# Making the taps' exponentials on GpSimd as powers of e in a fused dynamic convolution and SwiGLU kernel

## Chip, cores and metric

The kernel runs on one core of a Trainium2 chip. The metric is the device time of one execution in microseconds; the median of several runs is taken. The engines are named TensorE (PE in the profile, PEld its weight loads), VectorE (DVE), ScalarE (ACT), GpSimd (POOL) and SyncE (SP, which here only starts transfers).

## What is computed

The input x is 4 sequences of 4096 tokens with 192 numbers each; weight_gen has 8 heads of 7 taps for every token. The taps are made into weights by a softmax over the 7, and each token becomes a weighted sum of itself and the six tokens before it. The result goes through a gated MLP of width 1536.

```python
w = weight_gen - np.max(weight_gen, axis=-1, keepdims=True)
w = np.exp(w)
w = w / (np.sum(w, axis=-1, keepdims=True) + 1e-09)
...
out = np.einsum('bshk,bskhg->bshg', w, x_unf)
...
rms = np.sqrt(np.mean(x * x, axis=-1, keepdims=True) + 1e-06)
xn = x / rms * rms_g
g = xn @ w_gate
silu = g * (1.0 / (1.0 + np.exp(-g)))
val = xn @ w_val
return (silu * val @ w_out).astype(np.float32)
```

## The kernel before

Each of the 128 partitions holds 128 successive tokens. The work goes in 32 tiles (TILES) of 4 tokens per partition (J), 512 tokens in all. A tile's hidden layer is 12 blocks f of 128 rows. fp32 products are made in three parts from a rounded and a remaining half (w_hi, w_lo; xT part 0 and 1; h_hi, h_lo).

The order on each engine is written out by hand, with semaphores between the engines. In tile T:

- TensorE runs block f's gate and value products into PSUM (L620), and every two blocks the output projection of the two before (L651, L655). In the middle of the tile (block 5, for tile 0 block 9: `turn_after`, L154) it transposes the next tile's normalised input (L588, L592).
- ScalarE makes silu of the gate (L410) and, when VectorE has made h = value x silu (L544), the rounded h_hi (L417). Between these stand the squares of the next tile (L367, blocks 0 and 1), the scaling by 1/rms (L374, blocks 2 and 3), and the rounding of the transposed input (L379, L381). ScalarE works in order: a late scaling holds the silu behind it, and a late silu holds VectorE and TensorE.
- VectorE makes h (L544) and h_lo (L562) of each block. Between these stand the 17 steps of the convolution two tiles ahead (`mix`, L458): 4 of softmax normalising (L185 to L190, 32 or 224 columns), and 13 products and additions of 768 columns (L201, L203). Lists `steps_first`, `steps_taps` and `steps_other` (L528 to L530) say how many go with each block.
- GpSimd makes two small instructions per tile (`inverse_rms`, L289): an add (L292), and 1/rms as a power with exponent -0.5 (L294), each on 4 columns. At the start it also makes a part of tile 0's convolution and all of tile 1's.
- SyncE loads the inputs, moves halves of the transposed input between partitions (xT<-xT, L251) and stores results.

The taps of all tiles lie in one SBUF tensor, 224 columns per tile (32 token-heads of 7). Those of tiles 0 to FIRST-1 (FIRST is 3) are loaded first, in two pieces (`FIRSTS`): their maximum and difference are `less_max` on VectorE (L443), their Exp `first_exps` on ScalarE (L334). The others come in one transfer and are treated in three pieces, tiles 3 to 7, 8 to 19 and 20 to 31 (`cuts`, L163). Piece n has its maximum (`rest_maxima`, L506) and its difference (`rest_subtract`, L512) between VectorE's blocks of tile n, and its Exp (`rest_exps`, L389) on ScalarE behind block 9 of tile n. Exp and Silu lie in different tables of ScalarE, so each of these Exps has an ACT_TABLE_LOAD before it and one behind it. VectorE waits for the first piece's Exp at tile 1 and for all of them at tile 3 (L554). VectorE, ScalarE, GpSimd and SyncE run most tiles in loops (Fori) of two tiles; TensorE's tiles are written out.

Of the kernel before, what the change touches and what calls it, by code (L numbers as in the profile page):

```python
# [1 line left out]

# [3 lines left out]
ALU = mybir.AluOpType  # L6
ACT = mybir.ActivationFunctionType
AX_X = mybir.AxisListType.X
# [8 lines left out]
def dynconv_swiglu(nc, x, weight_gen, w_gate, w_val, w_out, rms_g, out):  # L17
# [18 lines left out]
    SLOTS = D // DB  # L36
    HB = 4
    CHUNKS = ((0, 1, 2), (1, 0, 2))
    FIRST = 3
    FIRSTS = ((0, 1), (1, FIRST))  # L40
    assert D == 192 and 2 * DB == P and F % P == 0 and (S // TOK) * TOK == S and TILES % 2 == 0
    NORM, CONV = 4, 2 * K - 1
# [9 lines left out]
    with ExitStack() as ctx:  # L52
        def sb(name, shape, dt=F32):
            return ctx.enter_context(nc.sbuf_tensor(name, shape, dt))
# [31 lines left out]
        mean_sq = sb("mean_sq", [P, J])  # L86
        minus_half = sb("minus_half", [P, J])
        eps_rms = sb("eps_rms", [P, J])
        zero = sb("zero", [P, 1])
        inv_rms = sb("inv_rms", [P, J])  # L90

# [68 lines left out]
            return f if f <= xf else f + 1  # L160


        cuts = [FIRST, 8, 20, TILES]  # L163
        pieces = [slice(a * J * H, b * J * H) for a, b in zip(cuts, cuts[1:])]

        def main_to(t, part):

# [111 lines left out]
        @block.gpsimd  # L279
        def _(pool):  # L280
            nc.gpsimd.memset(ident[:], 0.0).then_inc(pool_steps, 1)
            nc.gpsimd.memset(minus_half[:], -0.5).then_inc(pool_steps, 1)
            nc.gpsimd.memset(eps_rms[:], EPS_RMS).then_inc(pool_steps, 1)
            nc.gpsimd.memset(zero[:], 0.0).then_inc(pool_steps, 1)
            pool.wait_ge(pool_steps, 4)
            nc.gpsimd.affine_select(out=ident[:], in_=ident[:], compare_op=ALU.not_equal, fill=1.0, base=0,
                                    pattern=[[-1, P]], channel_multiplier=1).then_inc(consts_done, 1)

            def inverse_rms(T):  # L289

                pool.wait_ge(squared, J * (T + 1))
                nc.gpsimd.tensor_tensor(mean_sq[:], sq_mean[:], eps_rms[:], ALU.add).then_inc(mean_done, 1)  # L292
                pool.wait_ge(mean_done, T + 1)
                nc.gpsimd.tensor_tensor(inv_rms[:], mean_sq[:], minus_half[:], ALU.pow).then_inc(rms_done, 1)  # L294

            for b in range(2):
                p = b * (S // TOK)
                if b == 0:
                    pool.wait_ge(halo_loaded, 32)
                    pool.wait_ge(consts_done, 1)  # L300
                else:

                    pool.wait_ge(pool_zeroed, b)
                nc.gpsimd.memset(x_first[p:p + 1, 0:PAD, :], 0.0).then_inc(pool_zeroed, 1)
            pool.wait_ge(first_mix, NORM0_DONE)
            pool.wait_ge(pool_zeroed, 2)
            pool.wait_ge(x_zeroed, B - 2)
            pool.wait_ge(xfirst_loaded[0], 16)
            for n in range(CONV):
                if n:  # L310
                    pool.wait_ge(pool_mix, n)
                conv_step(nc.gpsimd, n, x_first[:, 0:PAD + J, :], tap_w, y[:, 0, :, :], prod_pool, J0, J).then_inc(pool_mix, 1)
            inverse_rms(0)
            pool.wait_ge(first_mix, NORM1_DONE)
            pool.wait_ge(xfirst_loaded[1], 16)
            for n in range(CONV):
                pool.wait_ge(pool_mix, CONV + n)
                conv_step(nc.gpsimd, n, x_first[:, J:PAD + 2 * J, :], tap_w1, y[:, 1, :, :], prod_pool).then_inc(pool_mix, 1)

            for T in range(1, 5):  # L320
                inverse_rms(T)

            def turn(i, last=False):
                for t in range(2):
                    if not (last and t == 1):
                        inverse_rms(2 * i + t + 1)

            with pool.Fori(2, TILES // 2 - 1) as i:
                turn(i)
            turn(TILES // 2 - 1, last=True)  # L330

        @block.scalar
        def _(act):
# [52 lines left out]
            act.wait_ge(wo_loaded, 16)  # L386
            nc.scalar.activation(wo[:, :, 0, :], raw_out, ACT.Copy).then_inc(w_hi_done, 1)

            def rest_exps(n):  # L389
                act.wait_ge(rest_less, n + 1)  # L390
                nc.scalar.activation(taps[:, pieces[n], :], taps[:, pieces[n], :], ACT.Exp).then_inc(rest_exp, 1)  # L391

            def out_low(T):


                act.wait_ge(bank_left, J * FB * (T + 1))
                nc.scalar.activation(out_part, out_ps[:, :, D:2 * D], ACT.Copy).then_inc(out_part_done, 1)  # L397

            def tile(T, t, first=False, last=False, exps=()):
                xf = turn_after(T)  # L400
                squares_at, scales_at = (xf - 4, xf - 3) if first else (0, 1), (xf - 2, xf - 1) if first else (2, 3)
                for f in range(FB):
# [23 lines left out]
                    for at, n in exps:  # L426
                        if f == at:
                            rest_exps(n)
# [13 lines left out]
        def _(dve):  # L442
# [63 lines left out]
            def rest_maxima(n):  # L506

                if n == 0:
                    dve.wait_ge(taps_loaded, 16)
                nc.vector.tensor_reduce(tap_max[:, pieces[n]], taps[:, pieces[n], :], AX_X, ALU.max).then_inc(rest_max, 1)  # L510

            def rest_subtract(n):  # L512

                dve.wait_ge(rest_max, n + 1)
                cols = pieces[n]
                nc.vector.tensor_tensor(taps[:, cols, :], taps[:, cols, :],
                                        tap_max[:, cols].unsqueeze(2).to_broadcast([P, cols.stop - cols.start, K]),
                                        ALU.subtract).then_inc(rest_less, 1)

            def out_add(T, t, stored):  # L520
                dve.wait_ge(out_part_done, T + 1)
# [4 lines left out]


            steps_first = [0, 0, 2, 2, 0, 2, 2, 2, 2, 2, 2, 1]  # L528
            steps_taps = [2, 2, 2, 0, 2, 2, 2, 0, 2, 1, 1, 1]
            steps_other = [2, 1, 2, 2, 1, 1, 1, 1, 2, 1, 2, 1]  # L530
            assert sum(steps_first) == sum(steps_taps) == sum(steps_other) == MIX

            def tile(T, t, i, first=False, mixes=True, last=False):
                xf = turn_after(T)
                tops = isinstance(T, int) and T < len(pieces)
                steps = steps_first if first else steps_taps if tops else steps_other
                max_at, subtract_at = (1, 4) if first else (3, 7)
                for f in range(FB):
                    b = pair(t, step_of(f, xf))
                    if f == 2 and not first:  # L540
                        out_add(T - 1, 1 - t, None if isinstance(T, int) and T < 3 else 16 * (i - (1 - t)))
                    dve.wait_ge(silu_done, FB * T + f + 1)
                    dve.wait_ge(val_done, FB * T + f + 1)
                    nc.vector.tensor_tensor(h[:, f % 2, :], val_ps[:, b, :], silu[:, f % 2, :], ALU.mult).then_inc(h_done, 1)  # L544
                    if first and f == 0:
                        wo_low()
                    if mixes:
                        for n in range(sum(steps[:f]), sum(steps[:f + 1])):
                            if n == 0:

                                dve.wait_ge(x_loaded[t], 16 * (i + 1))
# [17 lines left out]
            tile(0, 0, 0, first=True)  # L569
            tile(1, 1, 0)  # L570
            tile(2, 0, 1)
            tile(3, 1, 1)
            with dve.Fori(2, TILES // 2 - 1) as i:
                tile(2 * i, 0, i)
                tile(2 * i + 1, 1, i)
            tile(TILES - 2, 0, TILES // 2 - 1, mixes=False)
            tile(TILES - 1, 1, TILES // 2 - 1, mixes=False, last=True)
            out_add(TILES - 1, 1, 16 * (TILES // 2 - 1))

        @block.tensor  # L580
# [148 lines left out]
```

## Time and profile before

| | us |
|---|---|
| median of 3 runs | 1323.94 (1322.46 to 1326.7) |
| profiled execution | 1322.03 |
| its span in the trace | 1320.2 |
| TensorE busy | 1277.4 (97%) |
| VectorE busy | 992.0 (75%) |
| ScalarE busy | 662.8 (50%) |
| GpSimd busy | 83.3 (6%) |

The profile is that of one execution. Busy time is the time in which an engine's instructions run; matmuls are pipelined, so a busy TensorE needn't be at its peak. Idle time of an engine is put down to what released it: in a row, "[4.91 <-ACT silu L410]" says that the engine sat idle for 4.91 us until ScalarE's silu was there. The granted clock is TensorE's, as a share of 2.4 GHz. Times in rows are us from the span's start unless ns are named.

### The profile page before, as it was taken

Reading aid. Unit: us, or ns where it says so; the run is one execution under the profiler, and the core shown is the slowest. Engines: PE = TensorE matmul, PEld = TensorE weight load, DVE = VectorE, ACT = ScalarE, POOL = GpSimd, SP = SyncE. Lnnn points to the kernel's source line nnn. Section 1 sums busy time; section 2 is a strip of 40 time slices with the busy share of each in tenths; the row PEclk is TensorE's granted clock in tenths of the full one; section 3 lists DMA queues with packets and bytes.
Section 4 is the critical chain, followed back from the end, with each engine's and each line's share of the span. In section 5 each row is a group of like instructions: output and inputs, shape, how many; then the busy total and the mean of one; then the engine's idle time right before and its main releaser. Section 6 shows DMA issues by size and latency. Waiting matters only on the chain.

```text
span 1320.2 us, 33644 instructions
## 1 busy us (share of the span) xinstructions
PE 1277.4 (97%) x13524; PEld 1260.1 (95%) x13524; DVE 992.0 (75%) x1441; ACT 662.8 (50%) x1427; POOL 83.3 (6%) x101
## 2 busy tenths in 40 slices
PE   3798999999999999999999999999999999999998
PEld 3687889999999999999999999999999999999998
DVE  6788877777777778777778777777777777777653
ACT  4364565445555445555444555444555444555543
POOL 7600000000000000000000000000000000000000
PEclk9799999999999999999999999999999999999999
DMA  9121211211221211221211221111121121121010
GB/s 307 38 67 27 65 58 52 67 56 37 67 67 43 67 55 37 67 67 43 67 55 41 63 67 48 62 55 56 47 67 60 50 67 55 37 67 37 14 37 13
DMA packets 20101, 77.69 MB, mean 59 GB/s; under 512 B 3215, under 2 KB 5007, under 8 KB 19854
## 3 DMA queue, kind: packets, MB, share of 16 engines
q1 hardware_dynamic: 19982, 75.83, 18.9%
q8 instruction: 108, 1.77, 0.5%
q14 instruction: 11, 0.09, 0.0%
HBM read 38.07 MB, written 12.58 MB: 38 GB/s over the span
## 4 chain that ended last, share of the span: by engine, by line
PE 89%; DVE 5%; issue 2%; ACT 2%; DMA 1%; POOL 0%; SPq 0%; POOLq 0%
PE up_ps L620 59%; PE out_ps L651 26%; PE out_ps L655 3%; DVE y L203 1%; DVE h L544 1%; DVE h_lo L562 1%; DMA xT<-xT 1%; DVE prod L201 1%; PE up_ps L588 1%; ACT taps L391 0%; ACT silu L410 0%; PE up_ps L592 0%; DMA taps<-in_weight_gen 0%; ACT h_hi L417 0%; DVE y L201 0%
## 5 line engine op out<-in xcount | busy, mean ns | idle before, releaser
L620 PE MATMUL up_ps<-xT,w_hi 64*128 64x512 f32 x4608 | 858.1, 396 | 14.9 <-DMA xT<-xT 6.5
L620 PEld LDWEIGHTS up_ps<-xT,w_hi 64*128 64x128 f32 x4608 | 627.3, 186 | 26.1 <-issue 8.1
L620 PE MATMUL up_ps<-xT,w_lo 64*128 64x512 f32 x2304 | 589.2, 395 | 0.0
L651 PE MATMUL out_ps<-wo,h_hi 64*128 64x384 f32 x3072 | 478.2, 354 | 3.1 <-issue 2.7
L655 PE MATMUL out_ps<-wo,h_lo 64*128 64x192 f32 x3072 | 453.3, 247 | 0.0
L544 DVE TENSOR_TENSOR h<-up_ps,silu 128x512 f32<-128x512 f32 x384 | 264.7, 689 | 234.1 <-ACT silu L410 233.8
L651 PEld LDWEIGHTS out_ps<-wo,h_hi 64*128 64x128 f32 x3072 | 425.8, 185 | 5.1 <-issue 3.9
L655 PEld LDWEIGHTS out_ps<-wo,h_lo 64*128 64x128 f32 x3072 | 421.2, 187 | 0.5
L417 ACT ACTIVATE h_hi<-h 128x512 fp32r<-128x512 f32 x384 | 242.7, 632 | 352.3 <-DVE h L544 292.0
L410 ACT ACTIVATE silu<-up_ps 128x512 f32<-128x512 f32 x384 | 228.7, 595 | 263.7 <-PE up_ps L620 259.5
L620 PEld LDWEIGHTS up_ps<-xT,w_lo 64*128 64x128 f32 x2304 | 349.5, 187 | 3.3
L562 DVE TENSOR_TENSOR h_lo<-h,h_hi 128x512 fp32r<-128x512 f32 x384 | 265.2, 691 | 40.2 <-ACT h_hi L417 40.2
L203 DVE TENSOR_TENSOR y<-y,prod 128x768 f32<-128x768 f32 (+1 forms) x186 | 177.4, 954 | 2.1
L201 DVE TENSOR_TENSOR prod<-x_buf,tap_w 128x768 f32<-128x768 f32 x180 | 171.1, 951 | 1.5
L292 POOL TENSOR_TENSOR mean_sq<-sq_mean,eps_rms 128x4 f32<-128x4 f32 x32 | 8.2, 258 | 1149.2 <-ACT xn L367 1149.2
L374 ACT ACTIVATE xn<-y,inv_rms 128x128 f32<-128x128 f32 (+1 forms) x256 | 74.1, 360 | 4.4 <-POOL inv_rms L294 4.4
L525 DVE TENSOR_TENSOR last<-out_ps,last 128x768 f32<-128x768 f32 x32 | 30.6, 957 | 27.4 <-ACT last L397 27.4
L367 ACT ACTIVATE xn<-y 128x192 f32<-128x192 f32 x128 | 44.4, 348 | 1.6 <-DVE y L203 1.6
L294 POOL TENSOR_TENSOR inv_rms<-mean_sq,minus_half 128x4 f32<-128x4 f32 x32 | 34.0, 1064 | 2.5
L470 DVE TENSOR_TENSOR xT<-up_ps,xT 128x512 fp32r<-128x512 f32 x32 | 22.1, 691 | 10.7 <-ACT xT L381 9.2
L201 DVE TENSOR_TENSOR y<-x_buf,tap_w 128x768 f32<-128x768 f32 x30 | 28.7, 957 | 1.0
L473 DVE TENSOR_TENSOR xT<-up_ps,xT 64x256 fp32r<-64x256 f32 x64 | 26.6, 416 | 1.0
(43 smaller groups left out, 311.4 us busy)
## 6 DMA issues: line engine op xcount, KB each, us to landing
x_buf<-in_x SPq DMA_DIRECT2D x30, 960.0 KB, 4.5
xT<-xT SPq DMA_DIRECT2D x96, 256.0 KB, 3.8
result<-last SPq DMA_DIRECT2D x32, 384.0 KB, 2.3
taps<-in_weight_gen SPq DMA_DIRECT2D x1, 3248.0 KB, 19.5
raw<-in_moe_w_gate SPq DMA_DIRECT2D x3, 384.0 KB, 6.3
raw<-in_moe_w_val SPq DMA_DIRECT2D x3, 384.0 KB, 7.3
last<-in_moe_w_out SPq DMA_DIRECT2D x1, 1152.0 KB, 12.4
x_first<-in_x SPq DMA_DIRECT2D x2, 384.0 KB, 4.6
```

The lines of the kernel that those rows point to most:

```text
L201: return engine.tensor_tensor(heads(product if n else acc), heads(flat(src[:, k + j0:k + j1, :])), w[:, q0:q1, k].unsqueeze(2).to_broadcas ...
L203: return engine.tensor_tensor(acc, acc, product, ALU.add)
L294: nc.gpsimd.tensor_tensor(inv_rms[:], mean_sq[:], minus_half[:], ALU.pow).then_inc(rms_done, 1)
L367: nc.scalar.activation(xn[:, j * D:(j + 1) * D], y[:, t, j, :], ACT.Square, scale=D ** -0.5, accum_out=sq_mean[:, j:j + 1]).then_inc(squar ...
L374: nc.scalar.activation(part[:, j, :], y[:, t, j, d], ACT.Copy, scale=inv_rms[:, j:j + 1]).then_inc(xn_done, 1)
L410: nc.scalar.activation(silu[:, f % 2, :], gate_ps[:, b, :], ACT.Silu).then_inc(silu_done, 1)
L417: nc.scalar.activation(h_hi[:, f % HB, :], h[:, f % 2, :], ACT.Copy).then_inc(h_hi_done, 1)
L544: nc.vector.tensor_tensor(h[:, f % 2, :], val_ps[:, b, :], silu[:, f % 2, :], ALU.mult).then_inc(h_done, 1)
L562: nc.vector.tensor_tensor(h_lo[:, f % HB, :], h[:, f % 2, :], h_hi[:, f % HB, :].bitcast(F32), ALU.subtract).then_inc(h_lo_done, 1)
L620: mm = nc.tensor.matmul(ps[:, banks, :], w[rows, s, cols], xT[rows, t, s, part, :], start=(s == 0 and n == 0), stop=ends)
L651: nc.tensor.matmul(out_ps[:, j, 0:2 * D], h_hi[rows, g % HB, cols], wo[rows, g, :, :].rearrange("p a d -> p (a d)"), start=(g == 0 and k < ...
L655: mm = nc.tensor.matmul(out_ps[:, j, 0:D], h_lo[rows, g % HB, cols], wo[rows, g, 0, :], start=False, stop=(g == FB - 1 and k >= 2), skip_g ...
```

## The change

The taps of tiles 0 to 3 (FIRST is 4) keep ScalarE's Exp. For all others GpSimd makes the exponential as `pow` of a constant tensor filled with e and the differences, one instruction of 224 columns per tile. The maxima and differences on VectorE, before in pieces of 5 and 12 tiles, are made for tiles 4 to 7 in one go (maximum in tile 0 behind block 4, difference in tile 1 behind block 4), and from tile 8 on tile by tile, two tiles' worth in each of the tiles 3 to 14: maximum behind block 4 and difference behind block 6, and again behind blocks 7 and 9. GpSimd makes the powers of tiles 4 to 7 behind the inverse_rms it issues in tile 1, and two in each of the tiles 3 to 14 behind that tile's inverse_rms. VectorE waits for the power of tile T+2 before it normalises it in tile T. ScalarE has no table load between silus any more. The loops of VectorE, ScalarE and GpSimd are written out, and the list `steps_taps` goes (tiles 1 to 3 take `steps_other`).

```diff
-    FIRST = 3
+    FIRST = 4
...
+        euler = sb("euler", [P, J * H * K])
...
-        cuts = [FIRST, 8, 20, TILES]
-        pieces = [slice(a * J * H, b * J * H) for a, b in zip(cuts, cuts[1:])]
+        AHEAD = 8
+        def taps_at(T, f):
+
+            if T < 3 or f not in (4, 6, 7, 9):
+                return None
+            c = AHEAD + 2 * (T - 3) + f // 7
+            return c if c < TILES else None
...
+            nc.gpsimd.memset(euler[:], math.e).then_inc(pool_steps, 1)
+            pool.wait_ge(pool_steps, 5)
...
-            for T in range(1, 5):
-                inverse_rms(T)
...
+            def rest_exp_of(c):
+
+                pool.wait_ge(rest_less, c + 1 - FIRST)
+                w = taps[:, c * J * H:(c + 1) * J * H, :].rearrange("p q k -> p (q k)")
+                nc.gpsimd.tensor_tensor(w, euler[:], w, ALU.pow).then_inc(rest_exp, 1)
+
+            for T in range(TILES):
+                if T < TILES - 1:
+                    inverse_rms(T + 1)
+                if T == 1:
+                    for c in range(FIRST, AHEAD):
+                        rest_exp_of(c)
+                for f in (6, 9):
+                    c = taps_at(T, f)
+                    if c is not None:
+                        rest_exp_of(c)
...
-            def rest_exps(n):
-                act.wait_ge(rest_less, n + 1)
-                nc.scalar.activation(taps[:, pieces[n], :], taps[:, pieces[n], :], ACT.Exp).then_inc(rest_exp, 1)
...
-            tile(0, 0, first=True, exps=((9, 0),))
-            tile(1, 1, exps=((9, 1),))
-            tile(2, 0, exps=((9, 2),))
-            tile(3, 1)
-            with act.Fori(2, TILES // 2 - 1) as i:
-                tile(2 * i, 0)
-                tile(2 * i + 1, 1)
-            tile(TILES - 2, 0)
+
+            tile(0, 0, first=True)
+            for T in range(1, TILES - 1):
+                tile(T, T % 2)
...
-                                if isinstance(T, int) and T in (1, 3):
-
-                                    dve.wait_ge(rest_exp, 1 if T == 1 else len(pieces))
+                                if T + 2 >= FIRST:
+
+                                    dve.wait_ge(rest_exp, T + 3 - FIRST)
...
-                    if tops and f == max_at:
-                        rest_maxima(T)
-                    if tops and f == subtract_at:
-                        rest_subtract(T)
...
+                    if T == 0 and f == 4:
+                        rest_maxima(FIRST, AHEAD)
+                    if T == 1 and f == 4:
+                        rest_subtract(FIRST, AHEAD)
+                    c = taps_at(T, f)
+                    if c is not None:
+                        if f in (4, 7):
+                            rest_maxima(c, c + 1)
+                        else:
+                            rest_subtract(c, c + 1)
```

## Rows read from the trace of the kernel before

**Rows 1.** The page's first part: busy time, share of the span, instructions of each engine.
```profile
PE 1277.4 (97%) x13524; PEld 1260.1 (95%) x13524; DVE 992.0 (75%) x1441; ACT 662.8 (50%) x1427; POOL 83.3 (6%) x101
```

**Rows 2.** Stretches in us; busy us (instructions) by engine, PE's granted clock, DMA.
```profile
45.00:85.00 40.00, 36.03 (x372) 33.12 (x370) 35.47 (x45) 21.12 (x44) 12.19 (x7) 0.98 0.09 21
85.00:131.00 46.00, 42.37 (x428) 36.54 (x430) 37.09 (x49) 25.30 (x48) 1.21 (x2) 0.97 0.16 48
131.00:175.00 44.00, 40.41 (x420) 36.05 (x420) 34.67 (x46) 24.03 (x46) 1.21 (x2) 0.99 0.17 51
214.00:253.00 39.00, 39.00 (x421) 38.73 (x420) 30.08 (x45) 19.86 (x44) 1.21 (x2) 1.00 0.19 57
...
125.00:130.00 5.00, 3.13 (x28) 2.79 (x28) 2.74 (x5) 3.31 (x5) 0.00 (x0) 0.82 0.00 0
130.00:135.00 5.00, 5.00 (x46) 4.69 (x44) 3.34 (x7) 2.86 (x8) 0.00 (x0) 0.84 0.55 197
```

**Rows 3.** Timeline of ScalarE: start, us, instruction; silu of blocks 0 and 8, tiles 1-4.
```profile
86.57 0.60 ACT L410 ACTIVATE silu<-up_ps 128x512 f32<-128x512 f32 x1 [0.91 <-PE up_ps L620]
...
132.01 0.60 ACT L410 ACTIVATE silu<-up_ps 128x512 f32<-128x512 f32 x1 [1.33 <-PE up_ps L620]
...
160.86 0.60 ACT L410 ACTIVATE silu<-up_ps 128x512 f32<-128x512 f32 x1 [1.79 <-PE up_ps L620]
...
176.03 0.58 ACT L410 ACTIVATE silu<-up_ps 128x512 f32<-128x512 f32 x1
...
202.22 0.60 ACT L410 ACTIVATE silu<-up_ps 128x512 f32<-128x512 f32 x1 [2.40 <-PE up_ps L620]
...
215.26 0.60 ACT L410 ACTIVATE silu<-up_ps 128x512 f32<-128x512 f32 x1 [1.51 <-PE up_ps L620]
```

**Rows 4.** Timeline, the tenth block of tile 1: ScalarE, then VectorE behind it.
```profile
121.57 1.28 ACT L391 ACT_TABLE_LOAD   x1
122.86 2.45 ACT L391 ACTIVATE taps<-taps 128x2688 f32<-128x2688 f32 x1
125.33 1.28 ACT L410 ACT_TABLE_LOAD   x1
...
127.26 0.69 DVE L544 TENSOR_TENSOR h<-up_ps,silu 128x512 f32<-128x512 f32 x1 [4.91 <-ACT silu L410]
```

**Rows 5.** Groups by line and form, VectorE's differences: busy us, mean ns, idle before.
```profile
L516 DVE TENSOR_TENSOR taps<-taps,tap_max 128x2688 f32<-128x2688 f32 x2 | 5.9, 2952 | 0.0
...
L449 DVE TENSOR_TENSOR taps<-taps,tap_max 128x448 f32<-128x448 f32 x1 | 0.6, 624 | 0.0
```

**Rows 6.** Timeline: VectorE and TensorE in tile 3, ScalarE's scaling in tile 4.
```profile
190.97 0.68 DVE L562 TENSOR_TENSOR h_lo<-h,h_hi 128x512 fp32r<-128x512 f32 x1
191.59 0.69 DVE L544 TENSOR_TENSOR h<-up_ps,silu 128x512 f32<-128x512 f32 x1
...
197.85 0.68 DVE L562 TENSOR_TENSOR h_lo<-h,h_hi 128x512 fp32r<-128x512 f32 x1
...
193.43 0.45 PE L620 MATMUL up_ps<-xT,w_hi 64*128 64x512 f32 x2
...
223.65 1.16 ACT L374 ACTIVATE xn<-y,inv_rms 128x128 f32<-128x128 f32 x4
```

**Rows 7.** GpSimd's instructions: by line (ns min/median/max), then groups by form.
```profile
L294 POOL TENSOR_TENSOR inv_rms<-mean_sq,minus_half x32: 1007/1007/2471, 26.3 to 1242.1; 128x4 f32<-128x4 f32 x32
...
L292 POOL TENSOR_TENSOR mean_sq<-sq_mean,eps_rms x32: 198/200/1758, 24.5 to 1241.8; 128x4 f32<-128x4 f32 x32
...
L201 POOL TENSOR_TENSOR y<-x_first,tap_w 128x768 f32<-128x768 f32 x1 | 1.5, 1540 | 0.0
...
L201 POOL TENSOR_TENSOR y<-x_first,tap_w 128x192 f32<-128x192 f32 x1 | 0.7, 668 | 1.9 <-ACT x_first L346 1.9
```

**Rows 8.** Groups by form, VectorE's h_lo from 28 to 56 and from 204 to 243 us.
```profile
L562 DVE TENSOR_TENSOR h_lo<-h,h_hi 128x512 fp32r<-128x512 f32 x3 | 3.6, 1212 | 0.7 <-ACT h_hi L417 0.7
...
L562 DVE TENSOR_TENSOR h_lo<-h,h_hi 128x512 fp32r<-128x512 f32 x12 | 8.2, 686 | 0.7 <-ACT h_hi L417 0.7
```

More of the change, by code:

```diff
@@ L1 @@
+import math
 from contextlib import ExitStack
@@ L284, in _ @@
             nc.gpsimd.memset(zero[:], 0.0).then_inc(pool_steps, 1)
-            pool.wait_ge(pool_steps, 4)
+            nc.gpsimd.memset(euler[:], math.e).then_inc(pool_steps, 1)
+            pool.wait_ge(pool_steps, 5)
             nc.gpsimd.affine_select(out=ident[:], in_=ident[:], compare_op=ALU.not_equal, fill=1.0, base=0,
@@ L318, in _ @@
                 conv_step(nc.gpsimd, n, x_first[:, J:PAD + 2 * J, :], tap_w1, y[:, 1, :, :], prod_pool).then_inc(pool_mix, 1)
-            for T in range(1, 5):
-                inverse_rms(T)
[L323 to L330, printed above, removed]
+            def rest_exp_of(c):
[12 more added lines that the diff above has]
+                        rest_exp_of(c)
         @block.scalar
@@ L397, in out_low, with tile @@
                 nc.scalar.activation(out_part, out_ps[:, :, D:2 * D], ACT.Copy).then_inc(out_part_done, 1)
-            def tile(T, t, first=False, last=False, exps=()):
+            def tile(T, t, first=False, last=False):
                 xf = turn_after(T)
@@ L425, in tile @@
                         scale(T + 1, 1 - t, range(2 * n, 2 * n + 2))
-                    for at, n in exps:
-                        if f == at:
-                            rest_exps(n)
-            tile(0, 0, first=True, exps=((9, 0),))
-            tile(1, 1, exps=((9, 1),))
-            tile(2, 0, exps=((9, 2),))
-            tile(3, 1)
-            with act.Fori(2, TILES // 2 - 1) as i:
-                tile(2 * i, 0)
-                tile(2 * i + 1, 1)
-            tile(TILES - 2, 0)
+            tile(0, 0, first=True)
+            for T in range(1, TILES - 1):
+                tile(T, T % 2)
             tile(TILES - 1, 1, last=True)
@@ L504, in wo_low, with rest_maxima, rest_subtract @@
                                         ALU.subtract).then_inc(w_lo_done, 1)
-            def rest_maxima(n):
-                if n == 0:
+            def rest_maxima(c0, c1):
+                if c0 == FIRST:
                     dve.wait_ge(taps_loaded, 16)
[L510 to L515, printed above, removed]
+                cols = slice(c0 * J * H, c1 * J * H)
+                nc.vector.tensor_reduce(tap_max[:, cols], taps[:, cols, :], AX_X, ALU.max).then_inc(rest_max, c1 - c0)
+            def rest_subtract(c0, c1):
+                dve.wait_ge(rest_max, c1 - FIRST)
+                cols = slice(c0 * J * H, c1 * J * H)
                 nc.vector.tensor_tensor(taps[:, cols, :], taps[:, cols, :],
-                                        tap_max[:, cols].unsqueeze(2).to_broadcast([P, cols.stop - cols.start, K]),
-                                        ALU.subtract).then_inc(rest_less, 1)
+                                        tap_max[:, cols].unsqueeze(2).to_broadcast([P, (c1 - c0) * J * H, K]),
+                                        ALU.subtract).then_inc(rest_less, c1 - c0)
             def out_add(T, t, stored):
@@ L528, in _, with tile @@
             steps_first = [0, 0, 2, 2, 0, 2, 2, 2, 2, 2, 2, 1]
-            steps_taps = [2, 2, 2, 0, 2, 2, 2, 0, 2, 1, 1, 1]
             steps_other = [2, 1, 2, 2, 1, 1, 1, 1, 2, 1, 2, 1]
-            assert sum(steps_first) == sum(steps_taps) == sum(steps_other) == MIX
-            def tile(T, t, i, first=False, mixes=True, last=False):
+            assert sum(steps_first) == sum(steps_other) == MIX
+            def tile(T, t, first=False, mixes=True, last=False):
                 xf = turn_after(T)
-                tops = isinstance(T, int) and T < len(pieces)
-                steps = steps_first if first else steps_taps if tops else steps_other
-                max_at, subtract_at = (1, 4) if first else (3, 7)
+                steps = steps_first if first else steps_other
                 for f in range(FB):
@@ L540, in tile @@
                     if f == 2 and not first:
-                        out_add(T - 1, 1 - t, None if isinstance(T, int) and T < 3 else 16 * (i - (1 - t)))
+                        out_add(T - 1, 1 - t, None if T < 3 else 16 * ((T - 1) // 2))
                     dve.wait_ge(silu_done, FB * T + f + 1)
@@ L549, in tile @@
                             if n == 0:
-                                dve.wait_ge(x_loaded[t], 16 * (i + 1))
-                                if isinstance(T, int) and T in (1, 3):
-                                    dve.wait_ge(rest_exp, 1 if T == 1 else len(pieces))
+                                dve.wait_ge(x_loaded[t], 16 * (T // 2 + 1))
+                                if T + 2 >= FIRST:
+                                    dve.wait_ge(rest_exp, T + 3 - FIRST)
                             if n == NORM:
@@ L563, in tile @@
                                             ALU.subtract).then_inc(h_lo_done, 1)
-                    if tops and f == max_at:
-                        rest_maxima(T)
-                    if tops and f == subtract_at:
-                        rest_subtract(T)
[L569 to L577, printed above, removed]
+                    if T == 0 and f == 4:
[8 more added lines that the diff above has]
+                            rest_subtract(c, c + 1)
+            tile(0, 0, first=True)
+            for T in range(1, TILES):
+                tile(T, T % 2, mixes=T < TILES - 2, last=T == TILES - 1)
             out_add(TILES - 1, 1, 16 * (TILES // 2 - 1))
```

## The prediction

> **What bounds the kernel now.** I read the page's first part, then the stretches of single tiles, then the timeline of ScalarE and VectorE around the taps' exponentials. TensorE is busy 97% of the span, VectorE 75%, ScalarE 50%, GpSimd 6% [rows 1]. In the stretch of a settled tile TensorE is busy all of its 39 us [rows 2], and the first silu of one tile follows that of the tile before after 215.26 - 176.03 = 39.23 us [rows 3]. No edit at taps or engines beside TensorE shortens such a tile. What can be won lies ahead of 176 us: tile 1 takes 132.01 - 86.57 = 45.44 us and tile 2 takes 44.02 us [rows 3], with TensorE idle for 3.63 and 3.59 us in their windows [rows 2], so 6.2 and 4.8 us over a settled tile.
>
> Two things in these tiles differ from a settled one. (a) At the tenth block ScalarE leaves silu for a table load of 1.28 us, the Exp of 2.45 us and another load of 1.28 us, and VectorE waits 4.91 us for the next silu [rows 4]. (b) VectorE has a maximum and a difference of 2.95 us each [rows 5] between products. By silu starts in tile 2: its first eight blocks take 160.86 - 132.01 = 28.85 us against 202.22 - 176.03 = 26.19 in tile 3 [rows 3], so (b) costs 2.7 us and (a), in the last four, the other 2.1. In tile 1 (a) is some 3.5: there TensorE idles 1.87 us from 125 to 130 us, and the granted clock is 0.82 and then 0.84 in that stretch and the next [rows 2].
>
> **The change, part by part.**
> *ScalarE loses three Exps and six table loads.* They are the whole of (a): 3.5 + 2.1 = 5.6 us gained. In tile 0 no block of TensorE's is held by a silu then (the copies of the next tile's input come later anyway), so nothing there.
>
> *VectorE's large pieces go.* Tiles 1 and 2 lose their 2688-column maxima and differences, 2.7 us gained in each, 5.4. Tile 0 keeps a maximum (896 columns in place of 1120) and its difference moves to tile 1. The price per column is (2952 - 624) / (2688 - 448) = 1.04 ns [rows 5], so 1.09 us for 896 columns and about 1.5 us of VectorE's work leaves tile 0. TensorE idles 3.97 us of that window's 40 [rows 2]; between 0 and 1.5 us come back, I take 0.7. In tile 1 the 1.09 us difference stands right before block 5's product. In tile 3 that product ends at 191.59 + 0.69 = 192.28 and TensorE wants it at 193.43 [rows 6], so 1.15 us of cover for the product; the subtractions after the turn follow as late, and I charge 0.8 us (bounds 0 and the 2.7 of the old pieces).
>
> *VectorE's small pieces come.* In each of the 12 tiles 3 to 14 there are four more instructions of 224 columns, 0.39 us each by the slope, 1.6 us per tile. VectorE is busy 30.1 us of a settled tile's 39 [rows 2]. The one at block 4 fits in the 1.15 us above, the others fall where VectorE waits for silu. I charge nothing; the bounds are 0 and 12 x 0.4, if the cover of each turn were gone.
>
> *First loads.* Tile 3's taps now belong to the first Exp: 448 columns become 672, in VectorE's second maximum and difference, which stand ahead of its first convolution, and so ahead of everything. 2 x 224 x 1.04 ns = 0.47 us lost; the longer Exp and load wait for nothing, since ScalarE then waits for the convolution. The constant of e is one memset on an idle GpSimd. The loops of VectorE, ScalarE and GpSimd are written out; settled tiles show no idle TensorE, so neither a branch less nor more code fetched moves it (bounds 0 and some tenths).
>
> Sum, as long as GpSimd keeps up: -5.6 - 5.4 - 0.7 + 0.8 + 0.5 = -10.4 us.
>
> *GpSimd's power is the price that decides, and the trace doesn't show it at this size.* It shows a power of 4 columns at 1007 ns beside an add of 4 columns at 200 ns, and products of 192 and 768 columns at 668 and 1540 ns, 1.51 ns for each further column [rows 7]. Call p the time for a tile's 224 columns. From below: the 1007 ns are start, and 220 columns come at the product's rate, p = 1.3 us. From above: the 807 ns over the add are all work on four columns, 202 ns each, p = 1.0 + 220 x 0.202 = 45.4 us. The add's own 4-column row would give 50 ns per column, 33 times what the longer products show; so a rate read from 4 columns can be far too high. The middle in ratio is 7.8 us; I lean to the low side of it for that reason and take 5 us.
>
> What p may be before TensorE feels it. GpSimd works in order, so the powers of tile T stand ahead of inverse_rms of tile T+2, and ScalarE's scaling in block 2 of tile T+1 needs that, with silu queued behind it. In a settled tile the block-6 h_lo ends at 197.85 + 0.68, its small difference 0.39 later at 198.9, and scaling starts at 223.65 [rows 6]; less 1.2 us for the two inverse_rms instructions [rows 7] that leaves 23.5 us for two powers: p up to 11.7 costs nothing. The four powers in tile 1 start after block 4, in tile 3's times at 190.97 + 0.69 + 1.09 = 192.75, and have 29.7 us to the same point: p up to 7.4. Over that each late power shows whole:
> time = 1311.6 + (4p - 29.7, if positive) + 12 x (2p - 23.5, if positive).
>
> The sum is against the profiled execution's own 1322.03 us (its span is 1320.2, with 1.8 around it), which lies 1.9 us under the median of 1323.94. So 1311.6; against the median it would be 1313.5, and I say 1312.
>
> **A rule against a row.** While GpSimd runs the first convolutions VectorE's h_lo takes 1212 ns on average; afterwards, with GpSimd idle, 686 ns [rows 8]. The two engines slow each other here. By the Trainium skill, GPSIMD Engine Reference, Key points, GpSimd shares its SBUF interfaces with VectorE and contends with VectorE's instructions that have two SBUF inputs, and for elementwise work VectorE is about twice as fast. That agrees with the row and speaks against this change: by the rule each power slows VectorE while it runs, and it has its own rival below.
>
> **Rivals.**
> *GpSimd becomes the bound* (slower). Mechanism: inverse_rms queued behind two powers in tiles 3 to 14; it decides from p = 11.7 us (52 ns per column). p = 15 gives 1311.6 + 30 + 78 = 1420; p = 25 gives 1700; p = 45.4 gives 2271. For it: the 807 ns that four columns of power cost beyond four of an add. Against it: the factor of 33. Chance 0.32.
> *Half late*: p from 7.4 to 11.7, only the burst in tile 1 shows, up to 17 us: at p = 10 the time is 1322. Chance 0.13; under p = 8.9 still faster by over 0.3%, over 10.9 slower by as much.
> *VectorE slowed.* With p = 5 GpSimd is busy 10 of 39.2 us, a quarter. VectorE's h_lo and its 13 convolution steps take 12 x 0.69 + 13 x 0.95 = 20.6 us of a tile; a quarter of that lengthened by 77% is 4 us, beside 1.6 of new instructions, in 9 us of slack that isn't all where it is needed. If 1 us of it reaches TensorE per tile, 12 us are lost and the time is 1324: no change. For it: rows 8. Against it: a power does much between its reads, where a convolution step only streams. Chance 0.08.
> *It isn't the exponentials that cost tiles 1 and 2*, but their first passes through the code or the clock: then nothing comes back, 1322. Against it: the 4.91 us wait for silu right behind the table load. Chance 0.02.
>
> **How the numbers follow.** About 0.3%, 4 us, is what a measurement of this kernel can tell from no change. The forecast, p up to 7.4 with the gain whole, has 0.45, and its own range is 1306 to 1318 (its terms' bounds: T0's gain 0 to 1.5, tile 1's loss 0 to 2.7, small pieces 0 to 4.8). Faster: 0.45 and 0.04 of the half late case, 0.49. Same: 0.07 of half late, 0.06 of the slowed and 0.02 of the last rival, with 0.15 in all. Slower: the late GpSimd 0.32, 0.02 of half late and 0.02 of the slowed, 0.36. In the late case p may be anywhere from 11.7 to 45.4; half of it lies over 25 us, if spread by ratio. Leaving that half out (0.16) and a little at the low end puts the range at 1306 to 1700: wide, because one unseen price is.
>
> **What would show it.** In the profile after: the power's mean for 128x224, under 7.4 us; no table load after the first silu; tile 1 and 2 at 40 and 39.3 us from first silu to first silu; tiles 3 to 14 at 39.3; ScalarE's scaling never idle for GpSimd's inv_rms. I am wrong if scaling waits for inv_rms in block 2 of tiles 4 to 15 and those tiles take 15.8 + 2p us; if VectorE's h_lo rises over 0.8 us in tiles 3 to 14 with TensorE idle on it; or if tiles 1 and 2 keep their 45 us with the Exps gone.

## The result, and the profile after

| | before | after |
|---|---|---|
| median | 1323.2 us (4 runs, 1322.24 to 1326.7) | 2014.86 us (4 runs, 2012.12 to 2016.21) |
| span of the profiled execution | 1320.2 us | 2014.4 us |

The changed kernel takes 1.522 times as long (95% interval 1.520 to 1.524). The forecast was 1312 with a range from 1306 to 1700; the time lies outside it, on the side of the rival of a late GpSimd.

The page's first part, the chain's first line, and the groups of the power and the scaling (busy us, mean ns, idle before and who ended it):

```profile
PE 1301.1 (65%) x13524; PEld 1219.0 (61%) x13524; DVE 995.7 (49%) x1485; ACT 648.9 (32%) x1418; POOL 1093.6 (54%) x130
...
POOL 51%; PE 42%; DVE 3%; ACT 2%; DMA 1%; issue 1%; SPq 1%; ACTq 0%; POOLq 0%
...
L332 POOL TENSOR_TENSOR taps<-euler,taps 128x224 f32<-128x224 f32 x28 | 1011.0, 36125 | 195.2 <-DVE taps L518 195.2
...
L387 ACT ACTIVATE xn<-y,inv_rms 128x128 f32<-128x128 f32 (+1 forms) x256 | 74.1, 361 | 694.0 <-POOL inv_rms L302 694.0
```

TensorE does the same 13524 matmuls and is 65% busy where it was 97% [rows 1]. A power of 224 columns takes 36.1 us, and 28 of them 1011 us. ScalarE's scaling, which waited for GpSimd in tile 0 alone before, now waits 694 us for inv_rms, almost exactly the 692 us that the kernel lost. Where and how, in the timelines of GpSimd and ScalarE (start, us, instruction, idle before it), is seen in the burst of tile 1, then in a pair:

```profile
105.02 144.38 POOL L332 TENSOR_TENSOR taps<-euler,taps 128x224 f32<-128x224 f32 x4 [10.12 <-DVE taps L518]
249.37 0.20 POOL L300 TENSOR_TENSOR mean_sq<-sq_mean,eps_rms 128x4 f32<-128x4 f32 x1
...
376.40 1.01 POOL L302 TENSOR_TENSOR inv_rms<-mean_sq,minus_half 128x4 f32<-128x4 f32 x1
393.05 72.22 POOL L332 TENSOR_TENSOR taps<-euler,taps 128x224 f32<-128x224 f32 x2 [15.65 <-DVE taps L518]
465.24 0.20 POOL L300 TENSOR_TENSOR mean_sq<-sq_mean,eps_rms 128x4 f32<-128x4 f32 x1
...
250.69 1.17 ACT L387 ACTIVATE xn<-y,inv_rms 128x128 f32<-128x128 f32 x4 [103.34 <-POOL inv_rms L302]
...
377.44 1.17 ACT L387 ACTIVATE xn<-y,inv_rms 128x128 f32<-128x128 f32 x4 [48.98 <-POOL inv_rms L302]
```

The add of inverse_rms follows each group of powers with no idle time of its own: it has long been possible, but four powers (144.4 us) or two (72.2 us) stand ahead of it on GpSimd. ScalarE waits 103 us once and about 49 us twelve times; behind it in its order stands silu, so VectorE and TensorE wait too. From first silu to first silu the tiles take, in us (from ScalarE's timeline of each kernel):

| tile | 0 | 1 | 2 | 3 | 4 to 15 | 16 to 30 |
|---|---|---|---|---|---|---|
| before | 43.13 | 45.44 | 44.02 | 39.23 | 39.28 | 39.28 |
| after | 43.15 | 39.26 | 153.52 | 38.97 | 88.7 to 89.1 | 38.96 |

Tile 1 did get its 6.2 us back: no table load, no long piece. And there is a row that nobody had forecast: a settled tile takes 38.96 us, 0.32 less than before, though TensorE was never idle in one before [rows 2]. Both need an experiment, as does the question whether the power's length is all of the loss.

TensorE's granted clock falls too, from 0.992 over the whole kernel before to 0.825 here. Two stretches behind a wait (columns as in [rows 2]):

```profile
380.00:386.00 6.00, 6.00 (x40) 5.41 (x42) 5.80 (x9) 3.39 (x9) 0.00 (x0) 0.50 0.00 0
386.00:427.00 41.00, 36.00 (x382) 33.42 (x380) 25.00 (x40) 14.65 (x31) 33.95 (x1) 1.00 0.18 54
```

TensorE comes back at 379.96 us from 47 us of idleness, and its matmuls first run at 0.50 of the full clock, 1.2 GHz. From ScalarE's scaling to the next pair of powers the first pair has 14.54 us, at 1.00; the eleven later pairs have 15.24 to 15.62 us, with 0.50 in a part of it. So a late tile loses another 0.7 to 1.1 us beside the wait itself. The rows show the lower clock and the longer stretch together; no run changed the clock alone.

### The profile page after: what moved, and what is told of

Read it like the earlier page. It is cut to its first block, busy times and chain, and to the rows that moved or that the text cites. A ratio compares the mean times of both kernels' runs of the same rounds, so it can differ in the third digit from the quotient of the medians.

```text
span 2014.4 us, 32407 instructions
## 1 busy us (share of the span) xinstructions
PE 1301.1 (65%) x13524; PEld 1219.0 (61%) x13524; DVE 995.7 (49%) x1485; ACT 648.9 (32%) x1418; POOL 1093.6 (54%) x130
## 4 chain that ended last, share of the span: by engine, by line
POOL 51%; PE 42%; DVE 3%; ACT 2%; DMA 1%; issue 1%; SPq 1%; ACTq 0%; POOLq 0%
POOL taps L332 50%; PE up_ps L619 27%; PE out_ps L650 10%; PE out_ps L654 4%; DVE h L543 1%; ACT silu L419 1%; POOL inv_rms L302 1%; ACT xn L387 1%; DMA raw<-in_moe_w_val 1%; DVE prod L208 1%; DMA xT<-xT 1%; DVE h_lo L561 1%; PE up_ps L587 0%; DVE taps L518 0%; PE up_ps L591 0%
## 5 line engine op out<-in xcount | busy, mean ns | idle before, releaser
L619 PE MATMUL up_ps<-xT,w_hi 64*128 64x512 f32 x4608 | 810.1, 402 | 686.2 <-DVE h L543 677.4
L332 POOL TENSOR_TENSOR taps<-euler,taps 128x224 f32<-128x224 f32 x28 | 1011.0, 36125 | 195.2 <-DVE taps L518 195.2
L619 PEld LDWEIGHTS up_ps<-xT,w_hi 64*128 64x128 f32 x4608 | 497.6, 190 | 736.5 <-ACT silu L419 671.7
L619 PE MATMUL up_ps<-xT,w_lo 64*128 64x512 f32 x2304 | 487.6, 397 | 0.0
L650 PE MATMUL out_ps<-wo,h_hi 64*128 64x384 f32 x3072 | 465.1, 359 | 1.7 <-issue 1.2
L654 PE MATMUL out_ps<-wo,h_lo 64*128 64x192 f32 x3072 | 422.0, 249 | 0.0
L654 PEld LDWEIGHTS out_ps<-wo,h_lo 64*128 64x128 f32 x3072 | 331.3, 190 | 4.4
L650 PEld LDWEIGHTS out_ps<-wo,h_hi 64*128 64x128 f32 x3072 | 326.7, 187 | 6.5 <-issue 1.6
L619 PEld LDWEIGHTS up_ps<-xT,w_lo 64*128 64x128 f32 x2304 | 250.2, 191 | 22.1
```

The source lines that it names most:

```text
L332: nc.gpsimd.tensor_tensor(w, euler[:], w, ALU.pow).then_inc(rest_exp, 1)
L619: mm = nc.tensor.matmul(ps[:, banks, :], w[rows, s, cols], xT[rows, t, s, part, :], start=(s == 0 and n == 0), stop=ends)
L650: nc.tensor.matmul(out_ps[:, j, 0:2 * D], h_hi[rows, g % HB, cols], wo[rows, g, :, :].rearrange("p a d -> p (a d)"), start=(g == 0 and k < ...
L654: mm = nc.tensor.matmul(out_ps[:, j, 0:D], h_lo[rows, g % HB, cols], wo[rows, g, 0, :], start=False, stop=(g == FB - 1 and k >= 2), skip_g ...
```

## The experiments

The kernel before was run beside each on the same chip, with medians of 1322.8 to 1323.7 us.

**Is the power's length the whole loss?** The first kernel keeps everything but puts a product for the power:

```diff
-                nc.gpsimd.tensor_tensor(w, euler[:], w, ALU.pow).then_inc(rest_exp, 1)
+                nc.gpsimd.tensor_tensor(w, euler[:], w, ALU.mult).then_inc(rest_exp, 1)
```

> The changed kernel with GpSimd's power made a product of the same two operands (224 columns, so about 0.7 to 0.8 us in place of 36.1), everything else in place; the taps' exponentials of tiles 4 to 31 are left out by this. Theory (the power's duration is the whole loss, and the rest of the change gains what tiles 1 and 2 lost): no scaling waits for inv_rms, tiles 1 and 2 take 39.3 us each, total 1322.0 - 6.2 - 4.8 + 0.5 to 1.7 for a later start = 1312 to 1313. Rival (the small pieces on VectorE, the written-out loops, or GpSimd and VectorE at the same SBUF cost something too): over 1318, with TensorE idle in tiles 3 to 14.

Measured: 1303.35 us, ratio 0.985 (0.984 to 0.987). The product's 28 instructions take 724 ns on average, no scaling waits past tile 0, tile 1 takes 39.25 us. So the power's time, with the waits and the lower clock that come with it, is the whole loss, 711.5 us of it, and what is left of the change gains 20 us rather than 11. The settled tiles are again 38.96 us: 0.32 x 28 is the 9 us that neither theory had.

**Does the loss follow the queue?** The next two shorten the power, w[:, 0:112] and w[:, 0:56] in both operands and the output.

> The changed kernel with each power on the first 112 of its 224 columns; the other heads' exponentials are left out. From 1007 ns for 4 columns and 36122 ns for 224 a column costs 159.6 ns, so p = 18.2 us. Theory of the queue (inverse_rms behind the powers; each late power shows whole): 1312.8 + (4 x 18.2 - 29.7 = 43) + 12 x (2 x 18.2 - 23.5 = 12.9) = 1511 us, tiles 3 to 14 at 15.8 + 36.5 = 52.3 us each. Rival (the loss goes by GpSimd's total work against the span, or by VectorE's wait for the powers): 28 x 18.2 = 511 us of work fits in the span, so about 1313 to 1330.

> The changed kernel with each power on the first 56 of its 224 columns; the other heads' exponentials are left out. p = 0.37 + 56 x 0.16 = 9.3 us. Theory of the queue: two powers take 18.6 us of the 23.5 there are, so tiles 3 to 14 stay at 39.3 us; the burst of four in tile 1 takes 37.3 us of 29.7, so 7.6 us are lost in tile 2 alone: 1320.4 us. Rival (powers slow other engines while they run, in proportion to their time): VectorE's h_lo over 0.75 us in tiles 3 to 14, and a total over 1325.

The half: 1516.68 us. A power took 18.48 us, and with the base that the product kernel gave the rule says 1303.4 + (4 x 18.48 - 29.7 = 44) + 12 x (36.96 - 23.5 = 13.5) = 1509; tile 2 took 84.1 us (45.1 over a settled one) and tiles 4 to 15 between 52.4 and 53.4. The 8 us that the rule lacks are mostly in every second of these tiles, where 15.2 us pass from scaling to the power in place of 14.2; the granted clock is lowered in a part of both, and why they alternate is open. The rival, 1313 to 1330, is out: 517 us of power fit in the span but not in the queue. The quarter: 1312.13 us, ratio 0.992 (0.990 to 0.993), 8.8 us over the product kernel where the rule gives 4 x 9.3 - 29.7 = 7.5 (the 1320 that was expected lacked the faster pace). In the profiles 7.9 us of it are in tile 2 (46.86 us) and 1.4 in tile 0. Tile 0 takes from 43.1 to 45.9 us in the kernels of this document, with a granted clock of 0.97 in the shortest and 0.93 in the longest. Tiles 3 to 30 stay at 38.96. In its GpSimd timeline a pair of short powers leaves time before the next inverse_rms:

```profile
197.89 9.29 POOL L332 TENSOR_TENSOR taps<-euler,taps 128x56 f32<-128x56 f32 x1 [16.24 <-DVE taps L518]
207.38 9.28 POOL L332 TENSOR_TENSOR taps<-euler,taps 128x56 f32<-128x56 f32 x1 [0.20 <-DVE taps L518]
219.32 0.20 POOL L300 TENSOR_TENSOR mean_sq<-sq_mean,eps_rms 128x4 f32<-128x4 f32 x1 [2.66 <-ACT xn L380]
```

With the 2.66 us of idle time ahead of the add, the pair costs nothing; 260 us of power work are hidden but for the burst.

**What does a power cost?** Extra instructions behind the last inverse_rms, in the kernel before:

```diff
+            for c in (4, 8, 16, 32, 64, 112, 224):
+                pool.wait_ge(pw_done, done)
+                nc.gpsimd.tensor_tensor(pw_out[:, 0:c], pw_base[:, 0:c], pw_exp[:, 0:c], ALU.pow).then_inc(pw_done, 1)
...
+                nc.gpsimd.tensor_tensor(pw_sum[:, 0:c], pw_base[:, 0:c], pw_exp[:, 0:c], ALU.add).then_inc(pw_done, 1)
```

> The kernel before with extra instructions at the end of GpSimd's queue: powers and adds on 4, 8, 16, 32, 64, 112 and 224 columns (base e, exponent -0.75 everywhere), then powers of 64 columns with exponents -0.5, 0 and 2. Theory (a power's time goes by its columns, whatever the values): 0.37 + 0.16 us per column, so 1.0, 1.6, 2.9, 5.5, 10.6, 18.2 and 36.1 us, 10.6 for each of the three values; adds 0.2 us at 4 columns and about 0.5 at 224. Rival (small sizes have a start cost of their own, so 4 columns misled): 8 and 16 columns near 1.0 us. Rival (values matter): the exponents 0 and 2 take less than -0.75. The total time says nothing here, since the added work may pass the end.

GpSimd's groups by form, powers and adds:

```profile
L342 POOL TENSOR_TENSOR pw_out<-pw_base,pw_exp 128x224 f32<-128x224 f32 x1 | 36.5, 36462 | 0.1
L350 POOL TENSOR_TENSOR pw_out<-pw_base,pw_exp 128x64 f32<-128x64 f32 x3 | 31.6, 10545 | 0.2
...
L342 POOL TENSOR_TENSOR pw_out<-pw_base,pw_exp 128x64 f32<-128x64 f32 x1 | 10.6, 10558 | 0.1
...
L342 POOL TENSOR_TENSOR pw_out<-pw_base,pw_exp 128x32 f32<-128x32 f32 x1 | 5.4, 5439 | 0.1
L342 POOL TENSOR_TENSOR pw_out<-pw_base,pw_exp 128x16 f32<-128x16 f32 x1 | 2.9, 2899 | 0.1
L342 POOL TENSOR_TENSOR pw_out<-pw_base,pw_exp 128x8 f32<-128x8 f32 x1 | 2.2, 2173 | 0.1
L342 POOL TENSOR_TENSOR pw_out<-pw_base,pw_exp 128x4 f32<-128x4 f32 x1 | 1.0, 1007 | 0.1
...
L344 POOL TENSOR_TENSOR pw_sum<-pw_base,pw_exp 128x32 f32<-128x32 f32 x1 | 0.2, 250 | 0.1
...
L344 POOL TENSOR_TENSOR pw_sum<-pw_base,pw_exp 128x4 f32<-128x4 f32 x1 | 0.2, 198 | 0.1
```

A power takes (10558 - 5439) / 32 = 160 ns per column and some 0.3 us of start; of the 1007 ns at 4 columns 640 are work. The single row at 8 columns is half a microsecond above the line (0.3 + 8 x 0.16 = 1.6) and stays unexplained; an add of 64 columns stands out in the same way, 502 ns where 112 columns take 423. The values make no difference: exponents -0.5, 0 and 2 give 10545 ns, -0.75 gives 10558. An add from 4 to 32 columns costs (250 - 198) / 28 = 1.9 ns per column, and nearly all of its 198 ns is start.

**What were ScalarE's Exps worth, and who sets the pace?** In the kernel before, pieces 1 and 2 get a copy of one column in place of the Exp:

```diff
+                if n == 0:
+                    nc.scalar.activation(taps[:, pieces[n], :], taps[:, pieces[n], :], ACT.Exp).then_inc(rest_exp, 1)
+                else:
+                    nc.scalar.activation(zero[:], zero[:], ACT.Copy).then_inc(rest_exp, 1)
```

> The kernel before with the second and third late Exp (tiles 8 to 31) left out, a copy of one column in their place; so no table load in tiles 1 and 2, but VectorE's 2688-column pieces and the loops stay. The prediction's own terms give 5.6 us less than before, 1318. Theory of the pace (in the runs so far TensorE's settled tile is 38.96 us in place of 39.28, with nothing idle in either, and the waits at the table loads of tiles 1 and 2 are the last ones before the slower pace sets in): settled tiles at 38.96, so 9 us more, 1309. Rival (the written-out loops or VectorE's small pieces set the pace): settled tiles stay at 39.28, total 1318.

Measured: 1318.23 us against 1322.75, ratio 0.996 (0.995 to 0.998), 4.5 us. Tiles 1 and 2 take 41.80 and 41.81 us, so the Exps held 3.6 and 2.2 us in them. The total shows less of it because tile 0 took 1.5 us longer. The other 2.5 us of each go to VectorE's long pieces by what is left: they weren't taken out alone, but the last kernel below, which has neither Exps nor long pieces there, takes 39.28 in both tiles. The pace of settled tiles stays at 39.28: my theory that the last waits set it fell. So did the next suspicion:

```diff
-            with dve.Fori(2, TILES // 2 - 1) as i:
+            for i in range(2, TILES // 2 - 1):
```

(and so for ScalarE and GpSimd)

> The kernel before with nothing changed but the loops of VectorE, ScalarE and GpSimd written out. Theory of the pace set by the last waits: tiles 1 and 2 as before, settled tiles at 39.28, total as before, 1323 (ratio within 0.3% of 1). Rival (written-out loops give the faster pace): settled tiles at 38.96, total 1314.

Measured: 1323.87 us, ratio 1.0005 (0.9995 to 1.0014), pace 39.28. Loops or none, nothing changes.

What the five kernels at 38.96 so far shared (the changed one, the product, the half, the quarter, and the one with a power per tile, told below), and the four at 39.28 hadn't, was the constant of e: 896 bytes per partition in SBUF ahead of xn, xT and the h buffers. And the pace was there from tile 0 on: the 36 gate and value products of two blocks took 4.16 us with it and 4.22 without, from their first start to that of the projection behind them in TensorE's timeline. So the next kernel is the one before with an unused tensor there, and nothing else:

```diff
+        moved = sb("moved", [P, 224])
         zero = sb("zero", [P, 1])
...
+            nc.gpsimd.memset(moved[:], 0.0)
```

> The kernel before with one unused tensor of 224 columns (896 bytes per partition) in SBUF where the changed kernel has its constant of e, so that all tensors behind it (xn, xT, silu, h, h_hi, h_lo) lie 896 bytes further; one memset more, nothing else. Theory (the place of these tensors in SBUF sets TensorE's pace: all four kernels with the constant run 36 gate and value products in 4.16 us from tile 0 on, all four without it in 4.22): 4.16 us, settled tiles at 38.96, 0.32 x 31 = 10 us less, 1313. Rival (the pace comes with the written lists or the missing Exps): as before, 1323, 4.22 us.

Two smaller tensors in the same place, of 128 and of 288 bytes:

> The kernel before with the unused tensor of 32 columns, 128 bytes per partition. The kernel with extra powers had everything 3584 bytes (7 x 512) further and kept the slow pace; 896 bytes is 1 x 512 + 384. If the pace goes by the place within 256 bytes, 128 bytes do what 896 do: 4.16 us and 1313. If it goes by 512, something else may come out; if place doesn't matter, 4.22 and 1323.

> The same with 72 columns, 288 bytes per partition, another place within 256 (by 32) and within 512 (by 288). If the place within 256 bytes decides and 0 is slow, 128 fast, 32 should be nearer the slow one, 4.20 to 4.22; if any move gives the fast pace, 4.16.

Then the same 128 bytes put behind xT, ahead of silu:

> The kernel before with the unused 128 bytes between xT and silu, so that silu, h, h_hi and h_lo move and xT, the products' moving operand, stays. If xT's place decides: the slow pace, 39.28 us per settled tile, 1323. If the place of silu, h or the projection's weights decides: 38.96 and 1314.

| kernel | tensors from xn on | us | ratio to before (95%) | settled tile |
|---|---|---|---|---|
| moved by 896 | +896 (3 x 256 + 128) | 1314.02 | 0.993 (0.991 to 0.995) | 38.96 |
| moved by 128 (2 runs) | +128 | 1315.59 | 0.994 (0.992 to 0.996) | 38.96 |
| moved by 288 | +288 (256 + 32) | 1324.3 | 1.0007 (0.9996 to 1.0017) | 39.32 |
| extra powers | +3584 (14 x 256) | not comparable | | 39.28 |
| 128 behind xT | silu and on, xT not | 1324.12 | 1.0006 (0.9996 to 1.0015) | 39.29 |

The windows view over the same 400 us, kernel before, moved by 896, 128 behind xT (busy us of PE, PEld, DVE, ACT, POOL with instruction counts, granted clock, DMA share, GB/s):

```profile
600.00:1000.00 400.00, 400.00 (x4277) 400.00 (x4275) 309.45 (x459) 201.56 (x445) 12.08 (x20) 1.00 0.18 55
```

```profile
600.00:1000.00 400.00, 400.00 (x4316) 390.41 (x4314) 310.69 (x462) 203.27 (x451) 12.08 (x20) 1.00 0.20 58
```

```profile
600.00:1000.00 400.00, 400.00 (x4281) 387.48 (x4280) 309.38 (x459) 201.27 (x444) 12.07 (x20) 1.00 0.19 55
```

TensorE is busy all the time and at full granted clock in the three, yet gets 4316 matmuls done in place of 4277 or 4281. A share of busy time can't show this; the count per time, or the time between two like starts, does. Which of the tensors ahead of silu it is, xn or xT, wasn't tried apart; xT is the one that these products read. (The small tensors zero and inv_rms moved too, but TensorE reads neither.)

**Can the powers be had without the loss?** One power per tile rather than two, right behind an inverse_rms, with its difference made a tile earlier; tiles 3 to 7 keep the Exp of tile 0, which the kernel before has too. The lines that put this Exp back (FIRST is 3 again) and that move VectorE's pieces are left out here.

```diff
-            if T < 3 or f not in (4, 6, 7, 9):
+            if T < 1 or f not in (7, 9):
                 return None
-            c = AHEAD + 2 * (T - 3) + f // 7
+            c = AHEAD + T - 1
...
-                if T == 1:
-                    for c in range(FIRST, AHEAD):
-                        rest_exp_of(c)
-                for f in (6, 9):
-                    c = taps_at(T, f)
-                    if c is not None:
-                        rest_exp_of(c)
+                c = taps_at(T - 1, 9)
+                if c is not None:
+                    if T == 2:
+                        pool.wait_ge(rest_exp, AHEAD - FIRST)
+                    rest_exp_of(c)
...
```

> GpSimd still makes the powers of tiles 8 to 31 in full, but one per tile from tile 2 on, and each stands right behind an inverse_rms with its difference made a tile earlier: 1.2 + 36.1 = 37.3 us of the 39.0 between two inverse_rms. ScalarE makes the Exp of tiles 3 to 7 in tile 0 as in the kernel before. Nothing is left out. Theory (only the power's place in the queue ahead of inverse_rms costs, 36 us of work do not): no scaling waits for inv_rms, 1302 to 1304 as with the product, 1.5% faster than before. Rival (a GpSimd busy 95% of the time slows VectorE's instructions with two SBUF inputs, as its convolution did): h_lo over 0.75 us, settled tiles over 39.3, total over 1315. Rival (the powers run longer beside other work and pass the 39 us): scaling waits, over 1330.

Measured: 1303.46 us, ratio 0.985 (0.983 to 0.987), faster than both kernels. GpSimd's timeline, then VectorE's h_lo from 300 to 1000 us:

```profile
523.66 0.20 POOL L300 TENSOR_TENSOR mean_sq<-sq_mean,eps_rms 128x4 f32<-128x4 f32 x1 [1.57 <-ACT xn L378]
523.94 1.01 POOL L302 TENSOR_TENSOR inv_rms<-mean_sq,minus_half 128x4 f32<-128x4 f32 x1
524.92 36.14 POOL L332 TENSOR_TENSOR taps<-euler,taps 128x224 f32<-128x224 f32 x1
562.63 0.20 POOL L300 TENSOR_TENSOR mean_sq<-sq_mean,eps_rms 128x4 f32<-128x4 f32 x1 [1.57 <-ACT xn L378]
...
L563 DVE TENSOR_TENSOR h_lo<-h,h_hi 128x512 fp32r<-128x512 f32 x216 | 148.0, 685 | 11.3 <-ACT h_hi L424 11.3
```

24 full powers, 867 us of work, are hidden: inverse_rms starts when its squares are there, with 1.57 us to spare. And h_lo takes 685 ns beside a GpSimd that is busy 96% of the time, as in [rows 8] with an idle one.

Last, how much of this gain is the order of work and how much is the place in SBUF: the same kernel with the constant of e as the last tensor.

> The kernel with one power per tile a tile ahead, its constant of e now the last tensor in SBUF, so that xn, xT and all behind them lie where they lie in the kernel before. Theory (place in SBUF): the pace falls back to 4.22 us per 36 products and 39.28 per tile, 1303.5 + 31 x 0.32 = 1313. Rival (the pace belongs to the changed order of work): stays at 1303 to 1304.

Measured: 1313.05 us, ratio 0.992 (0.991 to 0.994), all settled tiles at 39.28. Half of the 20 us is the order of work, half is where xn and xT lie.

## Why the prediction was wrong

**What bounds the kernel, and what could be won** was right. Tiles 1 and 2 held 6.2 and 4.8 us over a settled tile. Of these the forecast gave (a), the Exps, 3.5 and 2.1, and (b), the long pieces, 2.7 each; the kernel without the late Exps shows 3.6 and 2.2, and 2.5 each. The rival that their first passes through the code or the clock held them is out. The sum of -10.4 us stands near what the last kernel measured, -10.5 (1313.05 against 1323.52), with its xT in the old place; but that kernel has another order of work, without the first loads and the piece in tile 1 that the sum charged. In the product kernel, which has all terms of the sum, the gain is 20.4 us, and 0.32 us for each of some 30 tiles leaves about 10.8. Single small terms are not confirmed: tile 0 took 43.13 us in both where 0.7 was to be gained, tile 1 ends 0.3 over the pace where 0.8 was charged, and the first silu came at 44.47 us in place of 43.44 where 0.5 was charged, a start that differs by half a microsecond among kernels that share it. So the agreement to 0.1 us is partly luck. The small pieces on VectorE cost nothing, as charged: settled tiles stay at the pace.

**The step that failed is the price p of the power.** The forecast took 5 us for 224 columns; the profile shows 36.1. The two bounds, 1.3 and 45.4 us, held it. The choice between them did not: "the add's own 4-column row would give 50 ns per column, 33 times what the longer products show; so a rate read from 4 columns can be far too high". That factor compares whole durations, and in an add of 4 columns nearly everything is start. But the upper bound had already taken the add's 200 ns away from the power's 1007. What was left, 807 ns, could only be work or a start that an add doesn't have, and the runs show 640 ns of work: 160 ns per column, against 202 in the bound. The same doubt was charged twice. The trace before couldn't say how much of the 807 was work, so it gave no ground for the low side either. With the whole excess read as work, the row of 4 columns gives 45.4 us for what took 36.1; as start it gives 1.3. The row of the same operation was the one to go by, not those of products of like size.

**The rival had the mechanism and its numbers.** With p = 36.12: 4p - 29.7 = 114.8 us, and tile 2 lost 153.52 - 38.96 = 114.6. 12 x (2p - 23.5) = 585 us, and tiles 4 to 15 lost about 49.9 each, 598. From the forecast's base that is 1311.6 + 700 = 2011, against 2014.86. Two misses are in this: the late tiles lost 13 us more than the rule gives, and the pace that was not foreseen took back 9 to 10. The period is 88.8 us where 15.8 + 2p gives 88.0, although each settled tile is 0.3 faster: the prediction took the distance from scaling to the next powers from a tile at full clock, and behind a wait, where TensorE starts at 0.50, it was some 15.3 us in place of 14.5. The 29.7 us of cover for the burst held in the kernel with 56 columns. Its chance, 0.32, was too small for a price that the trace gave at 4 columns, and the range to 1700 cut off the half of the case in which the price lay. (Two sums beside it are off: spread by ratio between 11.7 and 45.4 us, half of the case lies over 23 us, not 25; and the bounds given for the punctual case add up to 1310 to 1319, not 1306 to 1318. Neither would have brought 2015 into the range.)

**A wait that was not named.** With p = 36 the first power is also late for VectorE, which waits 12.4 us for it in tile 2 before it normalises. It costs nothing of its own, since inverse_rms is later still.

**VectorE slowed by GpSimd** did not come. The Trainium skill, SBUF — State Buffer, section Who interferes with whom, states that a VectorE instruction with two SBUF inputs contends with a GpSimd instruction that reads SBUF. The convolution's rows agree (1212 ns on average of three in place of 686 [rows 8]); a power, which reads two SBUF tensors too, shows nothing of it at 685 ns, so the measurement decides here. The prediction's remark that a power does much between its reads fits, and was not tested by itself; that the slowing goes by how often the instruction reads is a guess from these two cases.

**The written-out loops** cost nothing, as charged (1323.87 us with them alone). **The constant of e** was charged as one memset on an idle engine. Its 896 bytes moved everything behind it, and that was worth 9.5 us (1314.02 against 1323.52), more than the 5.8 us of the Exps in tiles 1 and 2.

## What to carry to other kernels

Price an instruction from the nearest row of the same operation, after its start is taken off by a cheap operation of the same shape; then don't discount it again. Better, time a second width first: 4 and 32 columns would have given (5439 - 1007) / 28 = 158 ns per column, and 35.8 us for 224. Work on a slow engine is free as long as nothing that another engine waits for stands behind it: put the long instruction right behind the short one that is due, one per period, and compute the period it must fit in. When a change adds or removes a buffer, compare the time of a settled stage in both kernels before crediting any other part; an unused tensor of the same size tells it.

## What the runs showed of the hardware

GpSimd's power of two tensors takes 160 ns per column of 128 fp32 and about 0.3 us of start, independent of the exponents tried, where its add takes about 2 ns per column. It doesn't slow VectorE's h_lo, which has two SBUF inputs: 685 ns beside a GpSimd that is busy 96% of the time. After 47 us of idleness TensorE's matmuls ran at a granted clock of 0.50 (380 to 386 us) before it was 1.00 again. TensorE's rate at full granted clock depends on where in SBUF a tensor from xn to xT starts: 36 products of 512 columns take 4.16 us with a move by 128 or 896 bytes, 4.21 to 4.22 with 0, 288 or 3584; the moves that help are 128 more than a multiple of 256. Why is open; the tensors' absolute addresses weren't read, and places other than 0, 32 and 128 within 256 weren't tried.
